# Expert blocks of sorted tokens in steps of 32 columns: ten TensorE code versions in place of three

## The chip, the cores and the metric

The kernel runs on one core of a Trainium2 chip. The metric is the device time of one execution in microseconds. A core has five engines that run side by side and meet through semaphores: TensorE (PE, matrix products), VectorE (DVE), ScalarE (ACT), GpSimd (POOL) and SyncE (SP). Each has a sequencer of its own that reads the engine's program, takes its branches and hands the instructions on. For PE the profile shows the sequencer's own instructions as `PEldq`, the weight loads as `PEld` and the products as `PE`.

## The reference, cut to what matters

```python
# x: (3072, 512), the output of a decayed linear attention (4 batches, 8 heads, 768 positions)
logits = x @ w_gate + modality_bias[modality_id]
e_idx = np.argmax(logits, axis=1)              # one of 8 experts for each token
gate_w = probs[np.arange(N), e_idx]
for e in range(E):
    mask = e_idx == e
    if not mask.any():
        continue
    h = np.maximum(x[mask] @ w1[e], 0.0)       # w1[e]: (512, 1024)
    out[mask] = gate_w[mask, None] * (h @ w2[e])   # w2[e]: (1024, 512)
# then a bilinear layer on all tokens
h = (out @ w1_) * (out @ w2_) @ w3
y = h @ w_out
```

Everything is float32. Worked out from this function and its default inputs, the tokens spread very unevenly: 1567 go to expert 0, 1502 to expert 3, 3 to expert 5 and none to the others.

## The kernel before

**Precision.** Each large product is made of three: operands are split in a high part (rounded to fp32r) and the rest, and high x high, high x low and low x high are summed in PSUM (`product`, L370). So 4 x 8 x 3 = 96 PE products make the hidden layer of a block, and 96 more its output.

**Stages.** First the attention with the gate's logits; then, while PE folds `w3 @ w_out` into `wc`, DVE works out each token's place in an order sorted by expert, and GpSimd scatters the rows to `x_sorted` in DRAM. Then come the expert blocks, which this case is about, and at the end six groups of 512 tokens through the bilinear layer.

**Expert blocks.** A block ("window") is up to 512 neighbouring rows of `x_sorted`, all of one expert. PE, ACT and DVE each run the loop `each_window`: NW = 13 rounds with the body skipped for rounds past the number of blocks (`num_tab`). For block `w`, PE reads from the table `win_tab` its size and which expert's weights it uses, takes the code version of that size, and runs `hidden` eight times (12 products each, into two PSUM banks by turns) and `outward` four times (24 products each). After each of the first two `outward` calls it transposes half of the next block's rows (`x_rows`, 8 transposes). The number of columns `n` of a product is a constant of the code, so each size has a full copy of the body: before there are three copies, of 4, 3 and 2 tiles of 128 columns, in this order in the program, inside nested `If`s. ACT and DVE have one body for all sizes: they always relu, split and copy 512 columns. The store of a block's output is 512 columns as well; a later block overwrites what was written past the end of an earlier one.

**The table.** `TILES` is the number of 128-row tiles of each expert, `WINS` how many blocks they need, and `SLACK` lets blocks be of 4 or 3 tiles. This is a chain of small DVE operations; each waits for the one ahead (`link`). It stands in DVE's order between the splits `wc_lo` and `w3_lo` that the fold of `wc` needs. The signal `s_tab` at its end is awaited by PE just before the first block, by GpSimd before its second load of `xin`, and by SP before the second expert's weights.

**Weights.** SP loads a new expert's weights into `we1_raw` and `we2_raw`; ACT and DVE split `we1` after the eighth hidden column group of the block before, and `we2` in the middle of the new expert's first block (after column groups 1 and 3).

**Hand-over.** During the last block ACT and DVE split the first inputs of the bilinear layer (`yT`, `wab`).

Of the kernel before, what the change touches and what calls it, by code (L numbers as in the profile page):

```python
# [24 lines left out]
ALU = mybir.AluOpType  # L25
ACT = mybir.ActivationFunctionType
AX = mybir.AxisListType
P = 128


def build(nc, q_t, k_t, k, v, mod_id, w_gate, mod_bias, we1, we2, wa, wb, w3_t, w_out, out):
# [18 lines left out]
    NW = (NI + 3 * E) // GT  # L50
    MINW = NT // GT
# [17 lines left out]
    def const(name, a):  # L69
# [9 lines left out]
                ("widx", every(np.arange(NW + 1))), ("gend", every(BANK * (np.arange(NG) + 1))), ("kidx", every(np.arange(E))),  # L79
                ("token", S * (np.arange(NT) % B) + P * (np.arange(NT) // B) + pos[:, None])]  # L80
# [11 lines left out]
    with ctx:  # L92
# [67 lines left out]
        e_sc = r("e_sc", [P, 11, E])  # L160
        e_int = r("e_int", [P, 2, E], I32)
        r = region(at_s + 16 * KB)
        w_sc = r("w_sc", [1, 6, NW + 1, E])
        w_k = r("w_k", [1, 5, NW + 1])
# [542 lines left out]
        def _(pe):  # L707
# [124 lines left out]
            def window(w, total):  # L832
                def wide(tiles):
                    run = table(pe, w, RUN_OF, 0, E - 1)
                    n = tiles * P
                    for f in range(KF):
                        hidden(w, run, n, f)
                    for d in range(KD):
                        outward(w, run, n, d)
                        if d < KD // 2:  # L840
                            with pe.If(total > w + 1):
                                x_rows(w + 1, range(2 * d, 2 * d + 2))
                size = table(pe, w, SIZE, 1, GT)
# [50 lines left out]
        def _(dve):  # L894
            chain = [0]

            def link(ins):

                chain[0] += 1
                ins.then_inc(s_v, 1)  # L900
                dve.wait_ge(s_v, chain[0])
# [119 lines left out]
            COUNT, TILES, CUM, USED, RUN, BASE, RUN1, WINS, PREV, SLACK, LAST = range(11)  # L1021
# [15 lines left out]
            def whole_tiles(dst, src, unit):  # L1037
# [5 lines left out]
            whole_tiles(row(TILES), row(COUNT), P)  # L1043
            link(ts(e_sc[:, TILES, 0:1], e_sc[:, TILES, 0:1], 1.0, None, ALU.max))
            whole_tiles(row(WINS), row(TILES), GT)
# [3 lines left out]
            link(ts(row(SLACK), row(WINS), -3.0, None, ALU.mult))  # L1049
            link(tt(row(SLACK), row(SLACK), row(TILES), ALU.add))  # L1050
            link(ts(row(USED), row(TILES), 1.0, None, ALU.min))
# [24 lines left out]
            past, mine, first, start, finish, tmp = (w_sc[:, i, :, :] for i in range(6))  # L1076
# [12 lines left out]
            link(tt(finish, finish, start, ALU.subtract))  # L1089
            link(tt(finish, finish, mine, ALU.mult))  # L1090
            link(dve.tensor_reduce(w_k[:, 0, :], finish, AX.X, ALU.add))
            link(ts(start, start, float(P), None, ALU.mult))
# [134 lines left out]
```

## Time and profile before

| | us |
|---|---|
| median of 3 runs (lowest to highest) | 906.22 (903.01 to 906.32) |
| the profiled execution, whole | 906.1 |
| its span, first to last instruction | 904.3 |
| PE products busy | 865.9 (96% of the span) |
| PE weight loads busy | 747.9 (83%) |
| DVE, ACT, POOL busy | 286.9, 239.6, 77.3 |

Read the stage first, then the engine. The expert blocks take from 182.3 to 503.6 us, a third of the span. There PE is busy nearly all the time, and ACT and DVE about a third. A pause of PE is told by what ended it: a semaphore of another engine, a DMA, or `issue`, in which case nothing of the other engines was late and one has to look at PE's sequencer. The instruction queues (`q8`, `q14`) among the DMA queues carry program code.

### The profile page before, as it was taken

The numbers are of one execution on the slowest core, as the hardware profiler recorded it, in microseconds if no ns is written. First come the engines' busy times: TensorE is split into PE (matmuls) and PEld (weight loads), VectorE is DVE, ScalarE is ACT, GpSimd is POOL, SyncE is SP. The second block draws the span as 40 slices with busy tenths as digits, with TensorE's granted clock in tenths as the row PEclk, the third lists the DMA queues.
The fourth block names the chain that finished last, engine by engine and source line by source line (L and its number), as shares of the span: only waits on it lengthen the run. The fifth ranks groups of instructions, "written<-read, shape, count | busy, mean of one in ns | idle before, by whom it ended". The sixth has DMA issues, their size and how long they took to land.

```text
span 904.3 us, 12985 instructions
## 1 busy us (share of the span) xinstructions
PE 865.9 (96%) x5028; PEld 747.9 (83%) x5029; DVE 286.9 (32%) x498; ACT 239.6 (27%) x388; POOL 77.3 (9%) x81
## 2 busy tenths in 40 slices
PE   6999999699899999999998999999999999999996
PEld 5989977578899998888888788888888888888884
DVE  2667778341212234121236232121121220230220
ACT  1223333231222243121236232122222221221210
POOL 2222016300000000000000001001001001001001
PEclk9999999899999999999999999999999999999998
DMA  9988754642120233111134101002002002001001
GB/s 328 307 280 283 267 203 171 189 151 81 48 89 6 93 139 139 47 46 46 46 139 165 68 1 70 24 0 82 12 0 81 12 0 93 0 0 46 1 1 46
DMA packets 42612, 85.93 MB, mean 95 GB/s; under 512 B 7120, under 2 KB 7632, under 8 KB 42576
## 3 DMA queue, kind: packets, MB, share of 16 engines
q1 hardware_dynamic: 30976, 56.13, 18.1%
q0 software_dynamic: 5744, 19.95, 6.1%
q10 hardware_dynamic: 5856, 9.33, 2.8%
q8 instruction: 27, 0.44, 0.2%
q14 instruction: 9, 0.07, 0.0%
HBM read 63.35 MB, written 22.04 MB: 94 GB/s over the span
## 4 chain that ended last, share of the span: by engine, by line
PE 78%; DMA 1%; issue 1%; ACT 0%; ACTq 0%; DVE 0%; POOL 0%; DVEq 0%; SPq 0%
PE bank L370 76%; PE pair L808 1%; DMA xin<-x_sorted 1%; DMA x_sorted<-x_keep,slot 0%; ACTq L319 0%; PE bank L808 0%; ACT we_p L533 0%; POOL out_dram L521 0%; ACT otile L533 0%; ACT yout L533 0%; ACT wc L533 0%; DVE hT L1135 0%; ACTq L619 0%; DVE we_p L918 0%; DVEq L319 0%
## 5 line engine op out<-in xcount | busy, mean ns | idle before, releaser
L370 PE MATMUL bank<-yT,wab 128*128 128x512 f32 x1152 | 262.2, 389 | 1.7 <-issue 1.7
L370 PEld LDWEIGHTS bank<-yT,wab 128*128 128x128 f32 x1152 | 216.1, 188 | 46.7 <-issue 1.9
L370 PE MATMUL bank<-xT,we_p 128*128 128x512 f32 (+2 forms) x768 | 154.0, 361 | 6.1 <-issue 2.6
L370 PEld LDWEIGHTS bank<-xT,we_p 128*128 128x128 f32 x768 | 136.6, 193 | 23.2 <-issue 5.0
L370 PE MATMUL bank<-hT,we_p 128*128 128x512 f32 (+2 forms) x768 | 153.4, 357 | 0.0
L370 PEld LDWEIGHTS bank<-hT,we_p 128*128 128x128 f32 x768 | 132.8, 188 | 14.4
L370 PE MATMUL bank<-wc,gT 128*128 128x512 f32 x576 | 131.5, 389 | 0.0
L370 PEld LDWEIGHTS bank<-wc,gT 128*128 128x128 f32 x576 | 108.1, 188 | 22.5
L1174 DVE TENSOR_TENSOR g<-bank,acopy 128x512 f32<-128x512 f32 x48 | 33.2, 692 | 258.8 <-PE bank L370 258.8
L1135 DVE SCALAR_TENSOR_TENSOR hT<-bank,hT 128x512 fp32r<-128x512 f32 x64 | 44.1, 691 | 165.6 <-ACT hT L609 165.6
L609 ACT ACTIVATE hT<-bank 128x512 fp32r<-128x512 f32 x64 | 38.2, 598 | 108.2 <-PE bank L370 108.2
L533 ACT ACTIVATE gT<-g 128x512 fp32r<-128x512 f32 x48 | 30.3, 632 | 136.6 <-DVE g L1174 136.6
L521 POOL DMA_INDIRECT out_dram<-otile,meta_in x24 | 23.2, 966 | 454.5 <-ACT otile L533 454.5
L533 ACT ACTIVATE yout<-bank 128x512 f32<-128x512 f32 x32 | 19.1, 597 | 114.4 <-PE bank L370 114.4
L370 PE MATMUL bank<-w_out_p,w3T 128*128 128x512 f32 x192 | 46.9, 404 | 1.9 <-issue 1.9
L533 ACT ACTIVATE acopy<-bank 128x512 f32<-128x512 f32 x48 | 28.7, 598 | 67.3 <-PE bank L370 67.3
L370 PEld LDWEIGHTS bank<-w_out_p,w3T 128*128 128x128 f32 x192 | 36.9, 194 | 10.4 <-issue 2.4
L918 DVE TENSOR_TENSOR gT<-g,gT 128x512 fp32r<-128x512 f32 x48 | 33.2, 693 | 33.9 <-ACT gT L533 33.9
L533 ACT ACTIVATE otile<-bank,meta_in 128x512 f32<-128x512 f32 x24 | 16.6, 690 | 100.0 <-PE bank L370 100.0
L918 DVE TENSOR_TENSOR xT<-pair,xT 128x512 fp32r<-128x512 f32 x30 | 19.3, 686 | 54.2 <-ACT xT L533 54.0
L718 PE MATMUL bank<-qkv 64*128 64x128 f32 x384 | 29.7, 297 | 4.5 <-DMA qkv<-in_q_t_dram 4.5
L744 PE MATMUL bank<-prob,qkv 128*64 128x128 f32 x384 | 28.0, 291 | 3.5 <-DVE prob L937 3.5
(128 smaller groups left out, 535.2 us busy)
## 6 DMA issues: line engine op xcount, KB each, us to landing
we_raw<-in_moe_w_dram SPq DMA_DIRECT2D x6, 2048.0 KB, 9.3
yT_sorted<-yout ACTq DMA_DIRECT2D x8, 1024.0 KB, 4.2
xin<-x_sorted POOLq DMA_DIRECT2D x7, 1024.0 KB, 5.6
qkv<-in_q_t_dram SPq DMA_DIRECT2D x24, 256.0 KB, 3.1
qkv<-in_v_dram SPq DMA_DIRECT2D x24, 256.0 KB, 4.4
ytile<-yT_sorted SPq DMA_DIRECT2D x6, 1024.0 KB, 4.9
qkv<-in_k_t_dram SPq DMA_DIRECT2D x23, 256.0 KB, 4.0
qkv<-in_k_dram SPq DMA_DIRECT2D x20, 256.0 KB, 4.8
```

The source lines that it names most:

```text
L370: i = pe.matmul(out_, left(a), right(b), start=(first and n == 0), stop=(last and n == 2), **kw)
L521: pool.indirect_dma_start(out[:, :], bass.IndirectOffsetOnAxis(ap=meta_in[:, n, 0:1].bitcast(I32), axis=0), otile[:, n % 2, :], None).then ...
L533: copy = lambda o, i, **kw: act.activation(o, i, ACT.Copy, **kw)
L609: act.activation(hT[:, HI, f, :], bank[f % 2][:, :], ACT.Relu).then_inc(s_hhi, 1)
L718: i = pe.matmul(bank[2 + r][:, t], qkv[head_rows(r), b, KT, t], qkv[head_rows(r), b, QT, t], start=True, stop=True)
L744: i = pe.matmul(bank[5][head_rows(r), j * P:(j + 1) * P], qkv[:, b, V, h * D:(h + 1) * D], prob[:, r, j, :], start=(first and j == 0), sto ...
L808: i = pe.transpose(bank[x_bank(w, k)][:, t * P:(t + 1) * P], xin[:, t, k * P:(k + 1) * P], ident)
L918: tt(pair(LO), raw, pair(HI).bitcast(F32), ALU.subtract).then_inc(sm_, 1)
L1135: dve.scalar_tensor_tensor(hT[:, LO, f, :], bank[f % 2][:, :], 0.0, hT[:, HI, f, :].bitcast(F32), ALU.max, ALU.subtract).then_inc(s_hlo, 1)
L1174: tt(g32[:, f % 2, :], bank[2 + f % 2][:, :], acopy[:, f % 2, :], ALU.mult).then_inc(s_g, 1)
```

## The change

The size of a block is counted in units of 32 columns. An expert's tokens, rounded up to units, are dealt to its blocks so that they differ by one unit at most. PE has ten versions of the body: 1 unit (32 columns) and 8 to 16 units (256 to 512 columns); a size in between is rounded up. A binary tree of `If`s picks the version. In the table's chain `SLACK` and the `start`/`finish` pairs go, and a division by counting (`q_sc`, `e_q`) comes in. Everything else is as before: the number of blocks, the columns that ACT, DVE and the stores take, the group stage.

```diff
+    UNIT = 32
+    FULL = BANK // UNIT
+    TINY, WIDTHS = 1, range(FULL // 2, FULL + 1)
...
             def window(w, total):
-                def wide(tiles):
+                def wide(units):
                     run = table(pe, w, RUN_OF, 0, E - 1)
-                    n = tiles * P
+                    n = units * UNIT
...
-                size = table(pe, w, SIZE, 1, GT)
-                with pe.If(size > 3):
-                    wide(4)
-                with pe.If(size < 4):
-                    with pe.If(size > 2):
-                        wide(3)
-                    with pe.If(size < 3):
-                        wide(2)
+                size = table(pe, w, SIZE, 1, FULL)
+
+                def pick(widths):
+                    if len(widths) == 1:
+                        wide(widths[0])
+                        return
+                    half = len(widths) // 2
+                    with pe.If(size < widths[half]):
+                        pick(widths[:half])
+                    with pe.If(size > widths[half] - 1):
+                        pick(widths[half:])
+
+                pick([TINY, *WIDTHS])
...
-            for dst, up in ((start, 0.0), (finish, 1.0)):
-                link(ts(dst, first, up, 3.0, ALU.add, ALU.mult))
-                link(tt(dst, dst, per_e(SLACK), ALU.add))
-                link(ts(tmp, first, up, 4.0, ALU.add, ALU.mult))
-                link(tt(dst, dst, tmp, ALU.min))
-                link(ts(dst, dst, 0.0, None, ALU.max))
...
+            link(tt(q_sc[:, :, :], of(WINS).unsqueeze(2).to_broadcast(wide_q), sm["times"][one].unsqueeze(1).to_broadcast(wide_q), ALU.mult))
+            link(tt(q_sc[:, :, :], q_sc[:, :, :], of(UNITS).unsqueeze(2).to_broadcast(wide_q), ALU.is_le))
+            link(dve.tensor_reduce(each, q_sc[:, :, :], AX.X, ALU.add))
+            link(tt(left, each, of(WINS), ALU.mult))
+            link(tt(left, of(UNITS), left, ALU.subtract))
+            per_q = lambda a: a.unsqueeze(1).to_broadcast(wide)
+            link(tt(size, first, per_q(left), ALU.is_lt))
+            link(tt(size, size, per_q(each), ALU.add))
```

PE's program grows from 424,320 to 629,504 bytes. An instruction is 64 bytes, so that is from 6,630 to 9,836 instructions, or 458 for each of the seven added versions.

PE's program at the head of the block loop and the end of its first version. `num_tab` and `win_tab` are the tables, L311 to L313 (L317 to L319 after) the loop, L319 (L325 after) a table read, L844 to L849 (L856, L858 after) the tests of the size. Before:

```order
L311 TENSOR_LOAD num_tab
L311 ISA x2
L312 UNCONDITIONAL_BRANCH
L313 COMPARE_AND_BRANCH
L319 ISA
L319 TENSOR_LOAD win_tab
L319 ISA x2
L844 COMPARE_AND_BRANCH
L319 ISA
L319 TENSOR_LOAD win_tab
```

The same place after:

```order
L317 TENSOR_LOAD num_tab
L317 ISA x2
L318 UNCONDITIONAL_BRANCH
L319 COMPARE_AND_BRANCH
L325 ISA
L325 TENSOR_LOAD win_tab
L325 ISA x2
L856 COMPARE_AND_BRANCH x3
L325 ISA
L325 TENSOR_LOAD win_tab
```

Before, one test stands ahead of the 512-column body. After, three stand ahead of the 32-column body, and the first of them branches over five versions for every size of 12 units or more. PE's program where the second half of the tree begins, behind the version of 352 columns (after):

```order
L376 MATMUL bank<-hT,we_p 128x352 x48
L858 UNCONDITIONAL_BRANCH
L858 COMPARE_AND_BRANCH
L856 COMPARE_AND_BRANCH x2
L325 ISA
L325 TENSOR_LOAD win_tab
```

This is where sizes 12 to 16 arrive. The 384-column body follows at once; those of 416, 448, 480 and 512 columns lie one to four bodies further on, and the loop's foot (L318) lies behind the last.

## Rows read from the trace of the kernel before

**Rows 1.** The page: span, its first part, and the chain that ended last.

```profile
span 904.3 us, 12985 instructions
...
PE 865.9 (96%) x5028; PEld 747.9 (83%) x5029; DVE 286.9 (32%) x498; ACT 239.6 (27%) x388; POOL 77.3 (9%) x81
...
PE 78%; DMA 1%; issue 1%; ACT 0%; ACTq 0%; DVE 0%; POOL 0%; DVEq 0%; SPq 0%
```

**Rows 2.** PE by shape: count, busy us, mean ns, idle before.

```profile
L370 PE MATMUL bank<-xT,we_p 128*128 128x384 f32 x288 | 52.3, 342 | 2.7 <-issue 2.6
...
L370 PE MATMUL bank<-xT,we_p 128*128 128x256 f32 x96 | 13.9, 307 | 2.6 <-DVE hT L1135 2.6
...
L756 PE MATMUL bank<-qkv,kdk 128*64 128x64 f32 x320 | 13.7, 231 | 0.0
```

**Rows 3.** PE's instructions in order of time (start us, us), 250 to 660 us.

```profile
302.75 16.91 PE L370 MATMUL bank<-xT,we_p 128*128 128x384 f32 x96
...
337.90 21.96 PE L370 MATMUL bank<-xT,we_p 128*128 128x512 f32 x96
...
383.25 21.92 PE L370 MATMUL bank<-xT,we_p 128*128 128x512 f32 x96
...
473.86 3.03 PE L370 MATMUL bank<-xT,we_p 128*128 128x256 f32 x24
...
490.19 11.68 PE L370 MATMUL bank<-hT,we_p 128*128 128x256 f32 x96
503.60 43.77 PE L370 MATMUL bank<-yT,wab 128*128 128x512 f32 x192 [1.73 <-issue]
```

**Rows 4.** The chain that ended last, in order of time: start us, us, what.

```profile
227.87 2.39 issue
230.26 22.64 PE bank L370 x120
...
267.14 0.25 issue
...
288.46 0.87 PE pair L808 x8
```

**Rows 5.** PE sequencer's branches by line: ns min/median/max, first to last start.

```profile
L846 PEldq COMPARE_BRANCH  x8: 73/148/3345, 223.7 to 471.8; - x8
...
L849 PEldq COMPARE_BRANCH  x4: 73/226/362, 263.9 to 472.2; - x4
...
L312 PEldq COMPARE_BRANCH  x13: 83/216/254, 227.2 to 503.4; - x13
```

**Rows 6.** DMA queues (packets, MB, share): code over the span; all, 275 to 500 us.

```profile
q8 instruction: 27, 0.44, 0.2%
...
q1 hardware_dynamic: 4736, 10.49, 13.2%
q10 hardware_dynamic: 2640, 5.24, 6.2%
q0 software_dynamic: 1088, 4.19, 5.6%
```

**Rows 7.** Stretches: us, busy by engine (count), then granted clock, DMA share, GB/s.

```profile
230.30:233.70 3.40, 3.40 (x12) 3.40 (x13) 0.00 (x0) 0.00 (x0) 0.00 (x0) 0.56 0.63 234
...
267.40:302.70 35.30, 35.30 (x208) 34.91 (x208) 8.11 (x12) 8.93 (x16) 0.75 (x1) 1.00 0.16 59
```

**Rows 8.** All engines in order of time in the last block.

```profile
479.60 2.36 DVE L918 TENSOR_TENSOR we_p<-we_raw,we_p 128x1024 fp32r<-128x1024 f32 x2 [1.07 <-ACT we_p L533]
...
482.62 7.74 PE L370 MATMUL bank<-xT,we_p 128*128 128x256 f32 x48 [2.34 <-DVE hT L1135]
...
489.36 0.69 DVE L1135 SCALAR_TENSOR_TENSOR hT<-bank,hT 128x512 fp32r<-128x512 f32 x1 [0.74 <-ACT hT L609]
```

**Rows 9.** Ahead of the blocks: the table chain's end, and PE's wait for rows.

```profile
149.24 0.16 DVE L1111 TENSOR_SCALAR need_tab<-need_k 1x6 int32<-1x6 f32 x1
...
176.74 1.97 PE L808 MATMUL bank<-small,xin 128*128 128x128 f32 x8 [8.81 <-DMA xin<-x_sorted]
```

More of the change, by code:

```diff
@@ L79, in build @@
                 ("widx", every(np.arange(NW + 1))), ("gend", every(BANK * (np.arange(NG) + 1))), ("kidx", every(np.arange(E))),
+                ("times", every(np.arange(FULL) + 1)),
                 ("token", S * (np.arange(NT) % B) + P * (np.arange(NT) // B) + pos[:, None])]
@@ L159, in build @@
         posf = r("posf", [P, NT])
-        e_sc = r("e_sc", [P, 11, E])
+        e_sc = r("e_sc", [P, 10, E])
         e_int = r("e_int", [P, 2, E], I32)
@@ L163, in build @@
         w_sc = r("w_sc", [1, 6, NW + 1, E])
+        q_sc = r("q_sc", [1, E, FULL])
+        e_q = r("e_q", [1, 2, E])
         w_k = r("w_k", [1, 5, NW + 1])
@@ L1020, in _ @@
             row = lambda i: e_sc[:, i, :]
-            COUNT, TILES, CUM, USED, RUN, BASE, RUN1, WINS, PREV, SLACK, LAST = range(11)
+            COUNT, UNITS, CUM, USED, RUN, BASE, RUN1, WINS, PREV, LAST = range(10)
             link(dve.tensor_copy(row(COUNT), cumt[:, :, NT - 1:NT].rearrange("p e n -> p (e n)")))
@@ L1035, in _, with whole_units @@
             wc_lo(0)
-            def whole_tiles(dst, src, unit):
+            def whole_units(dst, src, unit):
                 link(ts(e_int[:, 0, :], src, float(unit - 1), None, ALU.add))
@@ L1041, in whole_tiles @@
                 link(dve.tensor_copy(dst, e_int[:, 1, :]))
-            whole_tiles(row(TILES), row(COUNT), P)
-            link(ts(e_sc[:, TILES, 0:1], e_sc[:, TILES, 0:1], 1.0, None, ALU.max))
-            whole_tiles(row(WINS), row(TILES), GT)
+            whole_units(row(UNITS), row(COUNT), UNIT)
+            link(ts(e_sc[:, UNITS, 0:1], e_sc[:, UNITS, 0:1], 1.0, None, ALU.max))
+            whole_units(row(WINS), row(UNITS), FULL)
             scan = lambda dst, src: link(dve.tensor_tensor_scan(dst, sm["ones"][:, 0:E], src, 0.0, ALU.mult, ALU.add))
@@ L1048, in _ @@
             link(tt(row(PREV), row(CUM), row(WINS), ALU.subtract))
-            link(ts(row(SLACK), row(WINS), -3.0, None, ALU.mult))
-            link(tt(row(SLACK), row(SLACK), row(TILES), ALU.add))
-            link(ts(row(USED), row(TILES), 1.0, None, ALU.min))
+            link(ts(row(USED), row(UNITS), 1.0, None, ALU.min))
             scan(row(RUN1), row(USED))
@@ L1075, in _ @@
             per_w = sm["widx"][one].unsqueeze(2).to_broadcast(wide)
-            past, mine, first, start, finish, tmp = (w_sc[:, i, :, :] for i in range(6))
+            past, mine, first, start, size, tmp = (w_sc[:, i, :, :] for i in range(6))
             link(tt(past, per_e(CUM), per_w, ALU.is_le))
@@ L1082, in _ @@
             w3_lo(4)
-            for dst, up in ((start, 0.0), (finish, 1.0)):
-                link(ts(dst, first, up, 3.0, ALU.add, ALU.mult))
-                link(tt(dst, dst, per_e(SLACK), ALU.add))
-                link(ts(tmp, first, up, 4.0, ALU.add, ALU.mult))
-                link(tt(dst, dst, tmp, ALU.min))
-                link(ts(dst, dst, 0.0, None, ALU.max))
[L1089 to L1092, printed above, removed]
+            wide_q = [1, E, FULL]
+            each, left = e_q[:, 0, :], e_q[:, 1, :]
+            link(tt(q_sc[:, :, :], of(WINS).unsqueeze(2).to_broadcast(wide_q), sm["times"][one].unsqueeze(1).to_broadcast(wide_q), ALU.mult))
[6 more added lines that the diff above has]
+            link(tt(size, size, per_q(each), ALU.add))
+            link(tt(size, size, mine, ALU.mult))
+            link(dve.tensor_reduce(w_k[:, 0, :], size, AX.X, ALU.add))
+            link(ts(w_k[:, 4, :], w_k[:, 0, :], float(TINY), float(TINY - WIDTHS[0]), ALU.is_le, ALU.mult))
+            link(ts(w_k[:, 0, :], w_k[:, 0, :], float(WIDTHS[0]), None, ALU.max))
+            link(tt(w_k[:, 0, :], w_k[:, 0, :], w_k[:, 4, :], ALU.add))
+            link(tt(start, first, per_q(each), ALU.mult))
+            link(tt(tmp, first, per_q(left), ALU.min))
+            link(tt(start, start, tmp, ALU.add))
+            link(ts(start, start, float(UNIT), None, ALU.mult))
             link(tt(start, start, per_e(BASE), ALU.add))
```

## The prediction, made before the change was run

> **What bounds the kernel now.** I read the page's shares and the chain first: the chain is 78% PE, and PE is busy 96% of 904.3 us [rows 1]. So columns taken from PE's products are worth their time, where PE is not waiting. Then the list by shape and PE in order of time, to get a price per column. A block of 512 columns takes 383.25 - 337.90 = 45.3 us, one of 384 columns 337.90 - 302.75 = 35.2 us [rows 3]: 10.1 us for 128 columns, or 0.079 us for one. Transposes are not in this difference (8 take 0.87 us [rows 4]). The trace has eight blocks, of 512, 384, 384, 384, 512, 512, 512 and 256 columns, just what the default inputs give: expert 0 with 1567 tokens (13 tiles), expert 3 with 1502 (12), expert 5 with 3.
>
> Then I looked at PE's pauses between blocks, because the change multiplies the code there. Only one is large, 2.39 us of "issue" at 227.87, between the first block (512) and the second (384) [rows 2, 4]. No other engine was late. The sequencer's rows show the cause: one branch on L846 took 3.345 us, where a taken branch takes about 0.22 and one not taken 0.07 to 0.08 [rows 5]. It began at 223.7, 4.2 us before PE ran dry, so the sequencer works about 4 us ahead and that hid the rest. The code queue tells what it fetched: 27 pieces, 0.44 MB in all, so 16 KB or 256 instructions each [rows 6]. That is about PE's program (424,320 bytes) once over: nothing was fetched twice. From 275 to 500 us the code queue has no row at all [rows 6], while the loop went round five more times through three versions and its foot. So about 3 x 458 / 256 = 5.4 pieces were kept in the core. **The price of a branch to code that is not there is 3.345 - 0.22 = 3.1 us.** It has a second part: after the pause the granted clock is 0.56 for 3.4 us, the lower of the two levels (1.2 of 2.4 GHz) for most of it [rows 7], and that block took 36.9 us (230.26 to 267.14) instead of 35.3 [rows 4, 7]: 1.6 us more for each such pause.
>
> **The change, part by part.**
>
> *Fewer columns.* Expert 0 has 49 units in four blocks: 13, 12, 12, 12. Expert 3 has 47 in three: 16, 16, 15. Expert 5 has one. So the columns are 416, 384, 384, 384, 512, 512, 480, 32: 352 fewer, but only those of blocks 1 and 7 have the full price. Block 1: 96 x 0.079 = 7.6 us. Block 7: 32 x 0.079 = 2.5 us. Sum **-10.1**. No row has 416 or 480 columns; 96 products of 256, 384 and 512 columns take 11.68, 16.91 and 21.96 us [rows 3], near enough one line, so I take that line and no loss for odd widths.
>
> *The block of 32 columns.* It stands from 473.9 to 501.9, 28.0 us. Its 96 outward products take 11.68 us at 256 columns, 122 ns each [rows 3]. At 32 columns the weight load is what is left. The nearest row is the transposes, 128 columns on a full stationary, 0.87 / 8 = 109 ns [rows 4]: 96 x 0.013 = 1.2 us gained. The lowest row is 13.7 / 320 = 43 ns for 64 columns on a half stationary [rows 2], which would give 7.6. The hidden half is held by ACT and DVE, which still take 512 columns and split the new expert's weights there: PE waits 2.34 us for `hT`, two weight splits on DVE take 2.36 us, a relu split 0.69 [rows 8]. I give it 0.5. Sum **-1.7**, between 0 and -8.
>
> *The table chain.* As many DVE instructions as before, three of them on 128 elements instead of 112. It ends at 149.2 and PE then waits 8.81 us for the first rows at 176.7 [rows 9], which come from the scatter and not from the table. Queued behind the chain are the splits for `wc`; their lateness would end in that same wait. **0**, and up to 8.8 us late would still be 0.
>
> *More tests.* A pass through the tree costs one to three more tests and the branches over what is not taken, some 0.3 us at each of nine places (entry, seven changes of block, exit), partly within the sequencer's lead: **+2.5**.
>
> *Branches to code that is not there.* The body of the loop grows from 5.4 pieces to 10 x 458 / 256 = 17.9, or 293 KB. Its places lie far apart: head; second half of the tree, 8.9 pieces on, with 384 columns behind it; the bodies up to 512 columns, at the end; the foot. Each change of block needs the foot, the head and the middle, and for 13, 15 or 16 units a further test or body. No row shows how much can be kept beyond 5.4 pieces plus what follows them. Lower end: everything is kept and only the first visits cost. Entry has two (the middle, then the body of 416), the first foot one, the first 512 one or two, the exit none or one: 5. Upper end: nothing far away lives through a block: 31. I take that of three to four far places at a change about one is kept, which is the nearest to what the trace shows kept (a third of the new loop): **20 stalls**, so 20 x 3.1 = 62, less the one that is there already, **+59**. The pauses go from one to eight: 7 x 1.6 = **+11**. The lead hides about 1 us more than today at four places (blocks of 512 and the entry, where PE waits anyway): **-4**.
>
> Sum: -10.1 - 1.7 + 0 + 2.5 + 59 + 11 - 4 = **+57**. The profiled execution took 906.1 us (span 904.3), the median is 906.2, so they stand for each other: **963 us**.
>
> **What a page says.** The Trainium skill, page "Runtime: NRT & Kernel Launch", section "Instruction fetch mechanics", gives PE a store of 128 KiB refilled in blocks of 16 KiB and says that a taken branch to a target outside the current two pages forces a fetch before execution can go on. The piece size agrees with the trace (0.44 MB in 27); the two pages do not, since the loop ran over 5.4 pieces without a fetch. The 128 KiB would make the case in which all is kept less likely, and leave the forecast as it is.
>
> **The rivals.**
>
> *Each piece is fetched once* (5 stalls). For it: nothing was fetched twice before. Against: then all of 293 KB would have to be kept. 5 x 3.1 - 3.1 + 3 pauses x 1.6 + 2.5 - 2 - 11.8 = +6: **912 us** (908 to 920).
>
> *The code is there in time, and the columns win.* If the new versions' code were brought in during the sequencer's lead of 4 us, or kept from one pass on a path that ends at the same pieces, only today's stall would stay: 906.1 - 11.8 + 2.5 = **897 us**, faster. In its favour: every taken branch on L312, from the foot back to the head, took at most 0.254 us [rows 5]. Against it: the one first visit of a distant piece was a full 3.1 us and was not brought in ahead. It decides from the point where fewer than two stalls with their slow clock (4.7 us each) are added.
>
> *Every far branch stalls*, or a stall waits for the fetch ahead of it too. About 40 far branches at nine places: 40 x 3.1 = 124, less 3, and 11 + 2.5 - 4 - 11.8: +119, **1025 us**. The two-page rule above would do just this. For it: the foot's first visit stalled. Against: the same foot and head never stalled again.
>
> *The sizes do not come out as said.* If expert 0 had 50 to 52 units, block 1 would still be 416 columns and others would grow; the trace cannot tell, the inputs do. It moves the sum by under 7 us.
>
> **How the numbers follow.** Forecast, 925 to 1005 us: chance 0.70. Every far branch, above 1005: 0.10. Each piece once, 908 to 920: 0.13. Columns win, about 897: 0.07. The forecast's own ends are 10 stalls (31 - 3 + 8 + 2.5 - 3 - 11.8 = +24, 930; with the 32-column gain at its best 925) and 31 (+93, 999). Leaving out the two outer cases, 0.17, the range is **908 to 1005**. A difference under 0.5% (4.5 us) cannot be told from none; that takes the lower edge of the once-each case: faster 0.07, same 0.04, slower 0.89.
>
> **What would show each step right or wrong.** The code queue should have some 65 pieces or more instead of 27, with rows between 275 and 500 us. PE's chain should hold eight pauses of "issue" of 3 to 15 us at the changes of block, each with branches of 3.3 us on the size tests (L856, L858) and the loop's foot (L318), and a clock near 0.5 behind it. Block 1 without its pause should take 37.7 us, block 7 42.8, and the last about 26. If the code queue shows some 40 pieces and two or three pauses, the once-each case holds. If it shows many pieces but branches of 0.2 us, the price of a stall was wrong. If the blocks themselves take longer than these times, widths that are no multiple of 128 cost something that I left out.

## The result, and the profile after

The changed kernel took **1058.63 us** (median of 4 runs, 1056.37 to 1059.37), the kernel before, run beside it on the same chip, 906.27 us. The ratio is 1.168 (95% interval 1.164 to 1.172), or 152 us more. The forecast was 963 us with a range up to 1005, so it had the sign right and the size too small; the time lies beyond the rival "every far branch stalls" (1025 us), which had a chance of 0.10. The profiled execution has a span of 1054.4 us, 150.1 more than before. One of the twelve executions of the last version below ran at a mean granted clock of 0.75 and took 1089.71 us; its ratio is taken without that one.

The page of the changed kernel first: span, first part, the granted clock in 40 slices, the code queue, and the chain that ended last. They answer to [rows 1] and [rows 6].

```profile
span 1054.4 us, 13015 instructions
...
PE 889.4 (84%) x5028; PEld 776.0 (74%) x5029; DVE 286.4 (27%) x498; ACT 239.6 (23%) x388; POOL 75.3 (7%) x81
...
PEclk9999998898889886978969755999999999999998
...
q8 instruction: 100, 1.64, 0.8%
...
PE 69%; issue 13%; DMA 1%; ACT 0%; DVE 0%; POOL 0%; ACTq 0%; SPq 0%; DVEq 0%
```

PE's share fell from 96 to 84%, `issue` rose from 1 to 13% of the chain, and 100 pieces of code were fetched instead of 27. No other engine made PE wait longer in the blocks. The chain in order of time shows where: one long pause at the entry, at every change of block and at the exit. It answers to [rows 4] (start us, us, what).

```profile
179.50 11.26 issue
...
231.34 11.12 issue
242.46 22.57 PE bank L376 x120
...
279.30 15.44 issue
294.74 23.66 PE bank L376 x120
...
332.66 15.11 issue
...
384.83 24.46 issue
...
456.64 20.37 issue
...
524.58 15.89 issue
...
586.67 6.72 issue
593.39 41.13 PE bank L376 x192
634.52 17.79 issue
```

These nine sum to 138.2 us. Before, there were 4.5. Under them lie branches of PE's sequencer (ns min/median/max, first to last start), to set beside [rows 5]:

```profile
L318 PEldq COMPARE_BRANCH  x13: 76/3534/6587, 231.3 to 652.1; - x13
...
L856 PEldq COMPARE_BRANCH  x27: 65/3657/6572, 178.1 to 592.1; - x27
...
L858 PEldq COMPARE_BRANCH  x27: 68/80/5051, 184.7 to 638.7; - x27
```

Before, one branch of all these was slow. Now 31 take 3.3 to 6.6 us, 141 us together, 4.56 in the mean. At one change of block, between the two equal blocks of 384 columns, the rows of three slow branches in a row are these (the first line's maximum is the slow one, at 276.5):

```profile
L858 PEldq COMPARE_BRANCH  x2: 359/2672/4984, 276.0 to 276.5; - x2
...
L318 PEldq COMPARE_BRANCH  x1: 6318/6318/6318, 281.6 to 281.6; - x1
...
L856 PEldq COMPARE_BRANCH  x1: 4165/4165/4165, 289.1 to 289.1; - x1
```

So the end of the version, the loop's foot and the tree's test each waited for code, 15.5 us in all, and PE stood still for 15.44. This turn ran the same version as the one before it, and its code had still to be fetched again.

The second surprise is the block of 32 columns. It took 634.52 - 593.39 = 41.1 us instead of 28.0. PE in order of time, and the stretches (last three numbers: granted clock, DMA share, GB/s):

```profile
593.39 20.65 PE L376 MATMUL bank<-xT,we_p 128*128 128x32 f32 x96 [6.72 <-issue]
613.88 20.64 PE L376 MATMUL bank<-hT,we_p 128*128 128x32 f32 x96
...
600.00:610.00 10.00, 10.00 (x48) 10.00 (x49) 7.06 (x9) 5.67 (x8) 0.00 (x0) 0.50 0.06 8
610.00:620.00 10.00, 10.00 (x48) 10.00 (x48) 6.26 (x9) 5.87 (x10) 0.00 (x0) 0.50 0.61 225
620.00:634.50 14.50, 14.50 (x69) 14.41 (x68) 2.45 (x3) 2.97 (x4) 0.00 (x0) 0.50 0.16 58
```

A product of 32 columns took 215 ns at a granted clock of 0.50, the lower level of 1.2 GHz, all through the block. PE was busy without a gap, and the clock still did not rise.

The books over the span: pauses 138.2 - 4.5 = +133.6; the last block 41.1 - 28.0 = +13.1; blocks 1 to 7 without their pauses 293.5 instead of 288.9 = +4.6. That is +151.3, and -1.2 lies elsewhere. Versions below that run the new widths at the higher clock put the gain of the columns at 8.5 us (the forecast was 10.1), so +4.6 means about 13.1 us of slow clock behind the pauses. The rows agree: the first 96 products of the three blocks of 384 columns took 18.41, 19.50 and 18.64 us here, and 16.9 at the higher clock.

### The profile page after: what moved, and what is told of

Its sections match the earlier page's. It is cut to its first block, busy times and chain, and to the rows that moved or that the text cites. A ratio compares the mean times of both kernels' runs of the same rounds, so it can differ in the third digit from the quotient of the medians.

```text
span 1054.4 us, 13015 instructions
## 1 busy us (share of the span) xinstructions
PE 889.4 (84%) x5028; PEld 776.0 (74%) x5029; DVE 286.4 (27%) x498; ACT 239.6 (23%) x388; POOL 75.3 (7%) x81
## 3 DMA queue, kind: packets, MB, share of 16 engines
q1 hardware_dynamic: 30976, 56.13, 15.5%
## 4 chain that ended last, share of the span: by engine, by line
PE 69%; issue 13%; DMA 1%; ACT 0%; DVE 0%; POOL 0%; ACTq 0%; SPq 0%; DVEq 0%
PE bank L376 68%; PE pair L814 1%; DMA xin<-x_sorted 0%; DMA x_sorted<-x_keep,slot 0%; PE bank L814 0%; ACT we_p L539 0%; POOL out_dram L527 0%; ACT otile L539 0%; DVE hT L1153 0%; ACT wc L539 0%; ACTq L325 0%; DVE we_p L929 0%; ACT hT L615 0%; DVE wc L1005 0%; ACTq L609 0%
## 5 line engine op out<-in xcount | busy, mean ns | idle before, releaser
L376 PE MATMUL bank<-xT,we_p 128*128 128x384 f32 (+4 forms) x768 | 169.0, 384 | 121.5 <-issue 121.1
L376 PEld LDWEIGHTS bank<-yT,wab 128*128 128x128 f32 x1152 | 217.2, 189 | 63.1 <-issue 17.9
L376 PEld LDWEIGHTS bank<-xT,we_p 128*128 128x128 f32 x768 | 154.1, 222 | 136.7 <-issue 124.0
L376 PE MATMUL bank<-hT,we_p 128*128 128x384 f32 (+4 forms) x768 | 157.7, 362 | 0.0
L376 PEld LDWEIGHTS bank<-hT,we_p 128*128 128x128 f32 x768 | 141.8, 206 | 10.0
L376 PEld LDWEIGHTS bank<-w_out_p,w3T 128*128 128x128 f32 x192 | 37.7, 199 | 14.9 <-issue 6.9
```

The costliest lines, as they stand in the source:

```text
L376: i = pe.matmul(out_, left(a), right(b), start=(first and n == 0), stop=(last and n == 2), **kw)
```

## The experiments

The theory after this trace: PE's sequencer keeps about eight pieces of 16 KB of code, and when it fetches a piece the next one comes along. A loop that touches more than that fetches its code anew at each turn, and each jump to a piece that is not there waits. A simple model (eight places, the next piece fetched along, the one used longest ago makes room) run over the kernels' own instruction order gave the counts of the expectations; it was made to fit this trace, so only the kernels after it try it. A **slow branch** below is one over 2.2 us in the sequencer's rows. A time without an interval is that of a single execution; executions of the kernel before ranged from 901.6 to 910.2 us. A kernel with a jump table in place of the tree, for blocks of 8 to 16 units, gave no result, so what ten versions cost with one branch to each is not known.

### Are the widths to blame? Ten versions with the sizes of before

```diff
 # the kernel before, with the ten versions and the tree
...
+            link(ts(w_k[:, 0, :], w_k[:, 0, :], 2.0, 4.0, ALU.max, ALU.mult))   # the old sizes, as 8, 12 or 16 units
```

> The kernel before with the ten code versions and the tree of the change, but its own table: blocks of 512, 384, 384, 384, 512, 512, 512, 256 columns, so the same products as before. Theory (code that is not kept is fetched again and again): about 31 branches of 3.3 us or more, some 100 pieces in the code queue, 1045 to 1060 us. Rival (the new widths or the new table cost the time): near 906 us, 27 to 40 pieces.

**1064.12 us**, 103 pieces, 32 slow branches. The blocks are those of the kernel before, 512, 384 and 256 columns, and the whole loss is there. The widths are out; so is the new table.

### The 32-column block, apart from the code

```diff
-                    n = units * UNIT
+                    n = units * UNIT if units > TINY else BANK // 2
```

> The changed kernel, with 256 columns computed in the version for 1 unit; number of instructions and branches as in the change. Theory (products of 32 columns leave the clock at its lower level): last block back from 41.1 to about 28 us, total about 1045. Rival (the pauses around it keep the clock low): last block stays near 40 us, total about 1058.

```diff
 # the other way round, in the kernel before
-                    n = tiles * P
+                    n = tiles * P if tiles > 2 else 32
```

> The kernel before, with 32 columns computed in its smallest version in place of 256: no new code, no new branch. Theory (32 columns leave the clock low, each product then takes 213 ns): last block 41 us instead of 28, total about 919. Rival (as the prediction had it, the weight load at full clock): last block 26 us, total about 904.

The first took **1050.21 us**, the second **918.98 us** beside 906.21 for the kernel before: 12.8 us lost by computing 32 columns instead of 256. The first fell between its two totals (1045 and 1058), and its last block decides: it took 28.6 us (596.04 to 624.67), as before, while the pause behind it had grown from 17.79 to 20.57. So both runs fall on the side of the clock. The second kernel has one slow branch, so the effect doesn't hang on code. Its last block in order of time, and two stretches of it:

```profile
474.65 2.75 PE L370 MATMUL bank<-xT,we_p 128*128 128x32 f32 x24
...
493.66 20.64 PE L370 MATMUL bank<-hT,we_p 128*128 128x32 f32 x96
...
474.65:477.40 2.75, 2.74 (x25) 2.64 (x23) 0.20 (x1) 1.20 (x2) 0.00 (x0) 1.00 0.32 121
...
490.00:500.00 10.00, 10.00 (x48) 10.00 (x49) 6.13 (x9) 6.09 (x10) 0.00 (x0) 0.50 0.60 207
```

The first 24 products, right behind a block of 512 columns at the higher clock (1.00), took 2.75 us or 115 ns each. The 96 of the second half took 215 ns each at 0.50. So the estimate of 109 ns was right for the product and wrong for the clock that such products are run at.

### How many versions, and how far apart

Two kernels with fewer versions in the same tree:

```diff
-    TINY, WIDTHS = 1, range(FULL // 2, FULL + 1)
+    VERSIONS = [8, 12, 13, 16]        # and, in the other, [8, 12, 13, 15, 16]
```

> The changed kernel with four PE versions (256, 384, 416, 512 columns) in the same tree instead of ten; a block takes the smallest version that holds its units, so the blocks are 416, 384, 384, 384, 512, 512, 512, 256. PE's program is 453,632 bytes, a turn of the loop spans 7.3 pieces of 16 KB. Theory (PE keeps some 8 pieces and brings the next one along with a fetched one, so only a loop above that stalls): 4 to 6 slow branches, 36 to 40 pieces instead of 100, columns 7.6 us less, 5 stalls of 3.1 to 4.6 us partly hidden less the one of before, +2 us of clock: about 912 us (904 to 922). Rival (any branch over more than the 5.4 pieces of before stalls): two to three a turn, some 20 slow branches, 960 to 990 us.

> As the one with four versions, with a fifth of 480 columns (loop of 9.2 pieces; block 7 has 480 columns). Theory of the store: just above what is kept, so blocks that use the same versions again still find them, and the change to 512 columns starts to throw them out: 12 to 15 slow branches, 61 to 64 pieces, in the second half of the blocks; columns -10.1, stalls 13 x 4.6 - 3.1 = +57, clock +6: about 955 us (940 to 975). If the number of versions doesn't matter but the distance does, the same 20 stalls as with four versions. If the price is the number of tests, within 3 us of the one with four.

Four versions: **934.97 us**, ratio 1.031 (1.028 to 1.033), 45 pieces, 7 slow branches. Five: **967.69 us**, ratio 1.070 (1.068 to 1.073), 60 pieces, 15 slow branches. The one with five fell inside its bounds in time and slow branches and one piece below them. The one with four was 13 us above the upper end: seven slow branches instead of four to six, 45 pieces instead of 36 to 40, and pauses of 2.3 to 8.6 us behind them where I had allowed for hiding. The number of tests hardly differs, so the price is not the tests.

Next, distance against amount: all ten versions in the program, but tested one after the other with the three that run in front, and with the old sizes.

```diff
-                    half = len(widths) // 2
-                    with pe.If(size < widths[half]):
-                        pick(widths[:half])
-                    with pe.If(size > widths[half] - 1):
-                        pick(widths[half:])
-                pick([TINY, *WIDTHS])
+                    with pe.If(size == widths[0]):
+                        wide(widths[0])
+                    with pe.If(size != widths[0]):
+                        pick(widths[1:])
+                pick([FULL, 12, 8, TINY, 9, 10, 11, 13, 14, 15])
```

> Ten versions of code as in the changed kernel (629,504 bytes), but the sizes of the kernel before (512, 384, 384, 384, 512, 512, 512, 256) and another order of the versions: one test after the other, first 512, 384 and 256, then the seven that never run, so the code that runs lies in the first 5.4 pieces, and each turn jumps over 12.5 pieces to the foot and from there 18 back to the head. Theory of the store (what counts is how many pieces a turn touches): 2 to 4 slow branches and 31 to 34 pieces, about 912 us (907 to 920). Rival (how far a branch goes counts): at least two stalls a turn, 16 or more, 970 us or more. The same versions in the tree took 1064.1 us.

**922.73 us**, 33 pieces, 4 slow branches. With the tree the same ten versions and sizes took 1064.1 (above). The foot's row, where each turn jumps 18 pieces back to the head:

```profile
L315 PEldq COMPARE_BRANCH  x13: 83/221/5603, 228.3 to 518.0; - x13
```

Its median is 221 ns. So a far branch costs next to nothing if its target is kept, and of the 158 us that 293 KB of loop cost in the tree 17 are left if the turns touch few pieces of it. "Every far branch stalls" falls with this, though its price had come nearest. The time is 3 us above my bound; two of the four slow branches follow each other at the exit, a pause of 10.8 us. The second of them took 5.60 us; why is told below.

Which piece makes room?

```diff
-                pick([8, 12, 13, 16])   # tree
+                pick([13, 12, 16, 8])   # one test after the other
```

> The four versions of the 935.0 us kernel (416, 384, 512, 256 columns), the same blocks and the same program size (453,632 bytes), but one test after the other in the order in which they are needed instead of a tree. It tells which piece of the store makes room for a new one. If the one used longest ago: 12 slow branches and about 60 pieces, 955 to 965 us. If the one fetched longest ago: 6 slow branches and about 44 pieces, 925 to 938 us.

**969.4 us**, 60 pieces, 16 slow branches: as many pieces as the model where the one used longest ago makes room (four more slow branches than it has, and 4 us above my bound), and ten more slow branches than the model where it is the one fetched longest ago. That favours the first rule and does not prove it: the same model had missed the tree of four versions by nine pieces, and other rules and sizes of the store were not tried. An order that looks natural, by first use, is the worst of the four-version kernels.

### Is it the wait for code? A hint for the loop's back edge

```diff
-            with eng.Fori(0, NW) as w:
+            loop = nc.Fori(0, NW, engines=[mybir.EngineType.PE], hint_back_edge=True) if eng is nc.tensor else eng.Fori(0, NW)
+            with loop as w:
```

> The changed kernel with a prefetch hint for the loop's back edge on PE, at the top of each turn; nothing else. The eight slow branches from the foot of the loop to its head take 40 us of the 141 in the changed kernel. If the pauses are the wait for code and a hint brings the head's piece while the block runs, they fall to 0.2 us: 25 to 40 us less, 1020 to 1034 us. If the piece that is brought early is thrown out again before the foot, or the hint does nothing, 1055 to 1062 us, and then it says nothing about the cause.

**1000.73 us**: 58 us less by one instruction of 36 ns in each turn. The rows of the foot (L319 here) against L318 above, and the code queue:

```profile
L319 PEldq BRANCH_PREFETCH_HINT  x13: 31/36/55, 176.2 to 594.9; - x13
...
L319 PEldq COMPARE_BRANCH  x13: 87/234/3312, 231.1 to 595.5; - x13
...
q8 instruction: 65, 1.06, 0.5%
```

The hint changes nothing but when code is fetched, so the pauses that it took away were the wait for code. But it did more than I expected: 18 slow branches are left of 31, and 35 fewer pieces were fetched, where I had counted on the eight at the foot. Between the blocks of 384 columns no branch at all was slow any more (pauses 0.67 and 0.62 us instead of 15.44 and 15.11). Why a hint for one branch also keeps pieces for the others is open.

The hint in the kernels with four and five versions, and four versions with the tests in line and the much-used sizes first ([12, 16, 13, 8]):

> The kernel with four versions in a tree (935.0 us, 7 slow branches, 45 pieces) with the prefetch hint for the loop's back edge. In the changed kernel the hint took away 13 slow branches and 35 pieces, more than the eight back edges. If it works here as there, 2 to 4 slow branches are left, each pause 4 to 5 us: 905 to 922 us. If it serves only the back edge, one slow branch of seven goes: 928 to 933 us.

> The kernel with five versions in a tree (967.7 us, 15 slow branches, 60 pieces) with the same hint. If it works as in the changed kernel, 6 to 9 slow branches are left: 925 to 945 us. If it serves only the back edge, three slow branches of fifteen go (318 lines): 950 to 958 us.

> Four versions, one test after the other with those used by seven of eight blocks first (384, 512, 416, 256 columns), and the hint. A turn touches fewer pieces than in the tree (the tests stand next to the bodies). If the store of about eight pieces sets the time, 3 to 6 slow branches: 905 to 925 us; slower than before by 1% or more if each new expert's block still stalls once with its slow clock.

**929.27** (ratio 1.022, 1.018 to 1.025; 5 slow branches), **930.35** (1.024, 1.023 to 1.026; 6) and **912.90 us** (1.006, 1.005 to 1.008; 27 pieces, 3 slow). With four versions in the tree the hint took two slow branches of seven, the back edge's and one at the exit; with five it took nine of fifteen. The third fetches no piece twice. What it still loses is 9.0 us at the entry, where the first block's version stands third. So once more in order of first use, now with the hint:

> The four versions with the hint, one test after the other in the order in which they are needed first (416, 384, 512, 256 columns). The one with 384 and 512 ahead took 912.9 us with 27 pieces and three slow branches, two of them at the entry (a pause of 9.0 us) because the first block's version stood third. Here the first version stands right behind the first test: the entry's pause goes (-8), and in its place up to one slow branch each at the first 384, 512 and 256 columns (0 to 4 us each): 903 to 912 us. If the hint doesn't keep the pieces in this order (without it the same order had 16 slow branches and 969.4 us), 940 us or more.

> As the one before, with a fifth version of 480 columns ahead of that of 256 (10.1 us of columns less than before, not 7.6). With a store of eight pieces and a turn of 9.2 that touches few of them: 902 to 915 us. If five versions are too many even with the hint, slow branches at each change in the second half: 925 us or more.

**914.38 us** (1.010, 1.006 to 1.013; 29 pieces, 3 slow) and **934.94 us** (1.032, 1.028 to 1.037; 44 pieces, 9 slow). The entry's pause went, and three others of 3.3 to 4.1 us came: 2 us above my upper end. Five versions are too many even so; six of the nine slow branches are in one turn, ahead of the 256-column block, with a pause of 23.5 us.

### Why a slow branch behind another costs up to 6.6 us

```diff
                 with eng.If(total > w):
                     body(w, total)
+                if eng is nc.tensor:
+                    for _ in range(5):
+                        eng.value_load(num_tab[0:1, 1:2], min_val=MINW, max_val=NW)
```

> The changed kernel with five register loads (about 0.6 us each) on PE between the end of a block's code and the loop's back edge. In the changed kernel a slow branch that follows another one directly takes 4 to 6.6 us, one that stands alone 3.3 to 3.7. If it waits for the piece that the branch ahead of it let come along (two fetches in line), the slow branch of the back edge takes some 3 us less here (3.3 to 3.9 instead of 4.5 to 6.6 at turns 1 to 4 and 7), and the time stays within 5 us of 1058.6. If the longer time has another cause (the head is just slower to fetch), it stays at 6.2 to 6.6 us, and the kernel takes 15 to 25 us more, 1075 to 1085 us.

```profile
L318 PEldq COMPARE_BRANCH  x13: 76/3385/3960, 235.0 to 692.1; - x13
```

With 4.2 us of other work behind the slow branch ahead of it, the foot's branch took at most 3.96 us, where it had taken up to 6.59. The kernel took **1096.75 us**, more than either case said, since the loads were longer (up to 0.9 us, 4.2 for five) and are run in the five empty rounds too: the pause at the exit went from 17.79 to 36.47 us.

The code queue tells what the longer branches wait for, and there are two things. The first is another fetch of code beside their own. At the first turn the foot's branch took 4.86 us in the changed kernel, with two pieces fetched side by side (1.7 and 2.0 us), and 3.39 in the spaced one, where its piece came alone (0.9 us). The other piece need not come from a slow branch: at 276.5, 329.8 and 382.1 no slow branch is ahead, two pieces are fetched all the same, and the branches took 4.77 to 5.05 us; in the spaced kernel these three stay at 4.67 to 4.94.

The second is the data. In the three longest waits of the foot (6.17 to 6.59 us) no code at all was fetched for the first 2.1 to 2.6 us. The queues from the branch's start to its first fetch, and then to its end, for the one at 281.6 (packets, MB, share):

```profile
q10 hardware_dynamic: 415, 0.82, 98.8%
...
q8 instruction: 2, 0.03, 5.2%
```

`q10` carries the store of the block's output, 1 MB, and the fetches start when it ends. The wait of 6.57 us at the entry stands behind a 2 MB load of weights in the same way, and the one of 5.60 us at the exit of the kernel with ten versions in line behind a store. In all runs of this case 28 branches took over 5.1 us, four of them in the changed kernel; for each of them the fetch started 1.4 to 4.3 us after the branch where 1.0 us is usual, and data kept the DMA engines busy for 79% or more of that time. The spacing moved the foot's branch past the store as well as past the other fetch, so for the longest ones this run cannot tell the two apart, and the second cause is read from the rows alone: no run moved the store by itself.

### Where the sequencer's lead goes

In the versions in line the price of 3.2 to 3.5 us per slow branch is paid in full (pauses of 3.27 to 4.08 us), though the sequencer works 3.5 to 4 us ahead. The rows of the kernel before tell why. At the turn between blocks 2 and 3 the sequencer hands out its last product and starts the branch on L849 at 263.9 [rows 5], and the next block's first product starts at 267.39, just as PE runs dry (0.25 us of issue, [rows 4]). So the turn alone takes 3.5 us. (Behind a block of 512 columns the lead is longer: the slow branch of 3.35 us in [rows 5] left a pause of 2.39.) Two table loads and what belongs to them are a part of it:

```profile
L319 PEldq FUSED_REGOPS  x4: 51/103/151, 264.9 to 266.8; - x4
L319 PEldq TENSOR_LOAD <-win_tab x2: 302/304/307, 265.0 to 266.4; - x2
```

From the first of them to the end of the last one lie 264.9 to 267.0, with the tests in between. They can be read earlier, ahead of the last 24 products of a block:

```diff
+            def look_up(w):
+                for reg, col in ((next_size, SIZE), (next_run, RUN_OF)):
+                    pe.reg_load(reg, <win_tab, row w, column col>)
...
                     for d in range(KD):
+                        if d == KD - 1:
+                            look_up(w + 1)
                         outward(w, run, n, d)
...
-                size = table(pe, w, SIZE, 1, FULL)
+                size = nc.snap(next_size, engines=[PE_ENGINE], min_val=1, max_val=FULL)
```

> The kernel with four versions in order of use and the hint (914.4 us, three slow branches with pauses of 3.60, 4.08 and 3.27 us), with the two table loads of the next block (its size and run) moved from the turn of the loop to the middle of the last 24 products of a block. In the rows of PE's sequencer a turn of the loop without any slow branch takes 3.5 us from the last product's issue to the next block's first, as long as the sequencer's lead, so that a slow branch is added in full; the loads are 1.5 to 2.1 us of it. If that is so, each of the three pauses falls by 1.5 to 2 us: 914.4 - 3 x 1.7 - some clock = about 908 us (905 to 911). If the loads were hidden anyway, 913 to 916 us. With the columns' 7.6 us that would be a draw with the kernel before.

> The kernel before with the same two loads moved in the same way, nothing else. Its one pause at a change of block (2.39 us) falls to 0.3 to 0.9 us, with it a part of the slow clock behind it (1.6 us): 903 to 905 us, no more than measuring can tell. If the turn is hidden anyway, 906.

The first took **901.64 us**, ratio 0.995 (0.994 to 0.997), the second, the kernel before with nothing but this, **903.78 us**, ratio 0.997 (0.996 to 0.999). Both intervals lie below 1, by half a per cent and less. The pauses of the first, with the same three slow branches of 3.2 to 3.5 us as without it:

```profile
222.75 1.42 issue
...
259.53 2.01 issue
...
377.29 1.14 issue
```

They were 3.60, 4.08 and 3.27 us, so each fell by 2.1 to 2.2, or 6.4 together. The span fell by 11.5, from 910.8 to 899.3. The rest is the clock: the first 96 products of these blocks, without the early loads and then with them,

```profile
225.49 18.41 PE L377 MATMUL bank<-xT,we_p 128*128 128x384 f32 x96 [3.60 <-issue]
...
388.30 23.65 PE L377 MATMUL bank<-xT,we_p 128*128 128x512 f32 x96 [3.27 <-issue]
```

```profile
224.18 16.93 PE L377 MATMUL bank<-xT,we_p 128*128 128x384 f32 x96 [1.42 <-issue]
...
378.42 22.05 PE L377 MATMUL bank<-xT,we_p 128*128 128x512 f32 x96 [1.14 <-issue]
```

are as long as in [rows 3] again, 1.5 to 1.6 us less each, 4.6 for the three. The stretch behind the first of these pauses, without the early loads and with them, shows the clock:

```profile
225.50:229.00 3.50, 3.50 (x11) 3.50 (x12) 0.00 (x0) 0.00 (x0) 0.00 (x0) 0.53 0.22 84
```

```profile
224.20:228.00 3.80, 3.80 (x22) 3.80 (x23) 0.69 (x1) 0.60 (x1) 0.00 (x0) 1.00 0.71 276
```

Behind the pauses of 1.14 to 2.01 us the clock stayed at 1.00; behind those of 3.27 to 4.08 it was 0.53 to 0.62. Between them the length of the pause doesn't settle it: 2.39 us in the kernel before was followed by 0.56 [rows 7], 2.45 at the exit of this version by 1.00. With the clock the step was worth twice what I expected of it.

This version is ahead of both kernels of the case. Against the kernel before with the same early loads it is 2.1 us ahead in the medians, but the two intervals overlap (0.994 to 0.997 and 0.996 to 0.999), so that the finer blocks pay at all is not shown beyond the noise. In the traces the block of 416 columns is worth 6.9 us; the pauses take 3.7 back (7.0 us in all against 3.3), and this execution came to the blocks 1.8 us later.

| kernel | pieces | slow branches | us |
|---|---|---|---|
| before | 27 | 1 | 906.3 |
| changed: ten versions, tree | 100 | 31 | 1058.6 |
| ten, tree, old sizes | 103 | 32 | 1064.1 |
| ten, tree, hint | 65 | 18 | 1000.7 |
| ten in line, three used, old sizes | 33 | 4 | 922.7 |
| five, tree / with hint | 60 / 40 | 15 / 6 | 967.7 / 930.4 |
| four, tree / with hint | 45 / 37 | 7 / 5 | 935.0 / 929.3 |
| four in line by use, without / with hint | 60 / 29 | 16 / 3 | 969.4 / 914.4 |
| that with hint and early loads | 29 | 3 | 901.6 |
| before, with early loads | 27 | 2 | 903.8 |

## Why the prediction was right and wrong

**The step that failed is the one on branches to code that is not there.** The mechanism, its place (size tests and the loop's foot, at each change of block) and the look of the profile were as forecast. The term was "20 stalls" of 3.1 us, and both factors were too small. Of the 95 us that were missed, 76 lie in the pauses (+133.6 where stalls, tests and lead had +57.5), 15 in the block of 32 columns, and 4 in the rest.

- *The count.* 31 came, exactly my upper end ("nothing far away lives through a block"). I took two thirds of it, because the kernel before kept 5.4 pieces and a third of the new loop seemed to follow. That was an average where there is an edge. When room is made by dropping what was used longest ago, a loop a little larger than the store doesn't keep a share of itself; it keeps what it used last, which is what it needs last. Five versions show the edge: the entry and the first two turns cost four slow branches, the next turn none, the change from 384 to 512 columns one, and the turn after it, which runs 512 columns again, four.
- *The price.* 4.56 us in the mean, not 3.1. My one row of a slow branch [rows 5] was one that stood alone. Where a second piece of code is fetched beside the branch's own, it takes up to 5.1 us, and behind a large store or load of data up to 6.6. With 31 of 3.1 us the sum was 999 (its own terms give 997), still inside; 31 x 1.46 = 45 us on top carry it out of the range. The rival had the first half of this thought ("or a stall waits for the fetch ahead of it too") and gave it no price; the traffic of data was nobody's.
- *The lead covers -4.* It covered almost nothing: the 31 branches took 134.5 us more than as many quick ones of 0.22 would, and the pauses sum to 138.2. The turn uses the lead up. I read 4 us of lead from the rows and did not ask what else was in it.

**The block of 32 columns** was forecast at -1.7, between 0 and -8, and came at +13.1. I took 109 ns per product from the transposes, rows at the higher clock; the products stayed at the lower one. I had the clock as a price of pauses alone. The range should have looked above zero too: at half the clock the same rows give 192 x 0.218 = 41.9 us against 28.0, or +13.9.

**Right:** the sign, and the table chain (0): it ended at 150.2 instead of 149.2 with all ahead of it 1.1 us later, and PE still waited for the first rows, though for 1.14 us and not 8.81: mostly because its own straight code had a pause of 3.65 us there that I can't explain, with a clock of 0.50 behind it, and because the rows came 1.3 us earlier. **Nearly right:** the columns, forecast at -10.1, came at about -8.5. At the higher clock the block of 416 columns took 38.7 us (183.16 to 221.88 in the version in order of use with the hint) where I had 37.7, and 45.6 before; the block of 480 took 43.7 (431.96 to 475.62 in the one with five versions) where I had 42.8, and 45.3 before. The line between widths holds to 1.5%: 48 products of 384, 416 and 512 columns take 8.59, 9.29 and 11.14 us in the last version above, where a line gives 9.23 for 416, and 48 of 480 columns took 10.65 where it gives 10.50. The first block also waits 0.42 us for DVE's `hT`, which it did not at 512 columns.

Also nearly right: the clock behind pauses, forecast at 1.6 us for each of seven, came at 1.9; the stretch behind one of 11 us, and one of 15 us, in granted clock:

```profile
242.50:246.00 3.50, 3.50 (x12) 3.50 (x13) 0.00 (x0) 0.00 (x0) 0.00 (x0) 0.54 0.00 0
246.00:250.00 4.00, 4.00 (x25) 4.00 (x24) 1.38 (x2) 1.20 (x2) 0.00 (x0) 1.00 0.00 0
...
294.80:298.00 3.20, 3.20 (x10) 3.20 (x11) 0.00 (x0) 0.00 (x0) 0.00 (x0) 0.50 0.00 0
298.00:302.00 4.00, 4.00 (x18) 4.00 (x18) 0.69 (x1) 0.81 (x2) 0.00 (x0) 0.70 0.00 0
```

With the measured terms the sum reads 906.1 - 8.5 + 13.1 + (138.2 - 4.5) + 13.1 = 1057.5, and the profiled execution took 1056.4. It is no independent proof of the clock's 13.1, which is what was left over in the books.

The Trainium skill, page "Runtime: NRT & Kernel Launch", section "Instruction fetch mechanics", gives PE's store 128 KiB in blocks of 16 KiB, which is eight pieces; the runs fit about eight, with 36 to 40 pieces expected from it and 45 measured for four versions, and 61 to 64 and 60 for five. I had the figure and left the forecast as it was; had I let it set the count, 18 pieces of loop against eight, the upper end would have been the choice. The same section calls the store a FIFO and says that a taken branch to a target outside the current two pages forces a fetch. The run with four versions in order of use speaks against the first (60 pieces, as for the one used longest ago, against 44), and the median of 221 ns over 18 pieces against the second.

## What to carry to other kernels

- Before a loop's body is multiplied, count the code of PE that its turns touch, with the pieces between tests and foot and the one that comes along with each. A loop of 5.4 pieces of 16 KB fetched nothing again, one of 7.3 already did (45 pieces for a program of 28), and one of 17.9 fetched its code anew at every turn.
- Put the versions that run in turn next to each other, keep those that don't out of the way, hint the back edge, and take table reads out of the turn. A pause costs more than its length once the clock falls behind it: 6.4 us less of pause brought 4.6 us more in the products.
- Price a cost that comes in chains from a chain, not from the one case that stands alone, and ask of each hidden cost what already lies under the same cover. Look at what the DMA engines carry at that moment, too.
- Fewer columns pay only as long as the product keeps the clock high: 32 columns cost more than 256. Where between them it turns was not run.

## What the runs showed of the hardware that was not expected

- The runs fit a store of about eight pieces of 16 KB for PE's code that drops the one used longest ago and fetches the next along: four versions in a loop of 7.3 pieces 45 fetches, five (9.2 pieces) 60, ten (17.9) 100. At four versions it fetched more than such a store would (36 to 40 expected).
- A far branch to code that is not there takes 3.1 to 4.0 us when its piece is fetched alone, up to 5.1 with another piece fetched beside it, and up to 7.1 when its fetch starts behind a store or load of 1 MB or more (over all runs); 0.22 if the code is there, over any distance that was run.
- One prefetch hint on a loop's back edge (36 ns) took 58 us from the changed kernel.
- Products of 32 columns with a full stationary matrix ran at a granted clock of 0.50 for 41 us on end with PE busy throughout, 215 ns each, against 115 ns at the higher clock right behind wider ones.
